# Halo loads in two groups of partitions, low halves in other half steps, and the last two steps in natural order

## The reference

```python
w = np.exp(weight_gen - max); w = w / (sum(w) + 1e-09)          # [B, S, 8, 7]
x_unf = x_pad[:, np.arange(S)[:, None] + np.arange(7)[None, :], :]
out = np.einsum('bshk,bskhg->bshg', w, x_unf)
```

## Time and profile before

| | us |
|---|---|
| median of 3 runs | 1192.06 |
| lowest and highest run | 1190.22, 1192.4 |
| the profiled execution | 1188.5 |
| its span, first to last instruction | 1186.7 |
| PE busy | 1167.5 (98%) |
| DVE busy | 898.3 (76%) |
| ACT busy | 686.6 (58%) |

### The profile page before, as it was taken

The page is one execution under the profiler, slowest core; times in us unless marked ns, Lnnn a source line. Parts: engine busy times, 40 slices in busy tenths (PEclk is TensorE's granted clock), DMA queues, the critical chain, the costliest instruction groups (busy, mean ns, idle before and its releaser), DMA issues.

```text
span 1186.7 us, 26324 instructions
## 1 busy us (share of the span) xinstructions
PE 1167.5 (98%) x10808; PEld 1156.5 (97%) x10808; DVE 898.3 (76%) x998; ACT 686.6 (58%) x802; POOL 3.7 (0%) x11
## 2 busy tenths in 40 slices
PE   6999999999999999999999999999999999999998
PEld 6999999999999999999999999999999999999997
DVE  6888787786877878687786877868678786876564
ACT  5877655556555565555556555565555556555654
POOL 1000000000000000000000000000000000000000
PEclk9999999999999999999999999999999999999999
DMA  8312001010010100000010000100000010000000
GB/s 198 91 44 70 1 18 35 0 50 0 17 33 17 33 0 25 25 17 33 0 50 0 17 33 4 46 0 17 33 17 33 0 50 1 13 1 1 14 1 27
DMA packets 12816, 31.65 MB, mean 27 GB/s; under 512 B 1140, under 2 KB 7666, under 8 KB 12784
## 3 DMA queue, kind: packets, MB, share of 16 engines
q1 hardware_dynamic: 12784, 31.19, 8.4%
HBM read 24.89 MB, written 6.29 MB: 26 GB/s over the span
## 4 chain that ended last, share of the span: by engine, by line
PE 95%; DVE 2%; DMA 1%; ACT 1%; issue 1%; SPq 0%; DVEq 0%; ACTq 0%
PE h_ps L790 44%; PE y_ps L801 30%; PE y_ps L810 20%; PE y_ps L896 1%; DMA stage<-in_moe_w_out_dram 1%; DMA outs<-in_x_dram 1%; DVE acc L527 0%; ACT hid L362 0%; PE y_ps L903 0%; DVE hid_lo L607 0%; PE y_ps L909 0%; DVE prod L549 0%; DVE hid L596 0%; ACT hid L367 0%; ACT wout L349 0%
## 5 line engine op out<-in xcount | busy, mean ns | idle before, releaser
L790 PE MATMUL h_ps<-xt,win 64*128 64x512 f32 (+1 forms) x4860 | 1019.3, 379 | 0.3 <-DVE wout L580 0.3
L790 PEld LDWEIGHTS h_ps<-xt,win 64*128 64x128 f32 x4860 | 803.3, 185 | 0.8 <-DVE wout L580 0.5
L801 PE MATMUL y_ps<-hid_hi,wout 64*128 64x512 f32 (+1 forms) x2160 | 565.9, 381 | 1.3 <-DVE xt L588 1.2
L607 DVE TENSOR_TENSOR hid_lo<-hid,hid_hi 128x1024 fp32r<-128x1024 f32 (+1 forms) x270 | 313.1, 1160 | 173.8 <-ACT hid_hi L378 166.3
L378 ACT ACTIVATE hid_hi<-hid 128x1024 fp32r<-128x1024 f32 (+1 forms) x244 | 256.4, 1051 | 312.4 <-DVE hid L598 143.7
L801 PEld LDWEIGHTS y_ps<-hid_hi,wout 64*128 64x128 f32 x2160 | 370.1, 185 | 8.2 <-DVE xt L588 1.7
L810 PE MATMUL y_ps<-hid_lo,wout 64*128 64x512 f32 (+1 forms) x1080 | 327.5, 383 | 0.0
L801 PE MATMUL y_ps<-hid_lo,wout 64*128 64x512 f32 (+1 forms) x1080 | 322.8, 378 | 2.4 <-DVE hid_lo L607 2.3
L810 PE MATMUL y_ps<-hid_hi,wout 64*128 64x512 f32 (+1 forms) x1080 | 322.5, 378 | 0.0
L801 PEld LDWEIGHTS y_ps<-hid_lo,wout 64*128 64x128 f32 x1080 | 195.2, 185 | 3.0 <-DVE hid_lo L607 2.9
L810 PEld LDWEIGHTS y_ps<-hid_hi,wout 64*128 64x128 f32 x1080 | 195.1, 185 | 0.2
(11 more groups left out here) (70 smaller groups left out, 355.2 us busy)
## 6 DMA issues: line engine op xcount, KB each, us to landing
xwin<-in_x_dram SPq DMA_DIRECT2D x14, 960.0 KB
out_dram<-outs SPq DMA_DIRECT2D x16, 384.0 KB, 2.5
stage<-in_moe_w_out_dram SPq DMA_DIRECT2D x8, 384.0 KB, 6.4
stage<-in_moe_w_in_dram SPq DMA_DIRECT2D x4, 512.0 KB, 6.4
stage<-in_moe_w_in_dram SPq DMA_DIRECT2D x8, 256.0 KB, 6.2
wraw<-in_weight_gen_dram SPq DMA_DIRECT2D x16, 112.0 KB, 2.3
xwin<-in_x_dram SPq DMA_DIRECT2D x1, 768.0 KB
outs<-in_x_dram SPq DMA_DIRECT2D x2, 283.5 KB
```

Of the source, the lines that this page charges most:

```text
L607: dve.tensor_tensor(lo, hid[:, slot, :, 0:width], hi.bitcast(fp32), ALU.subtract).then_inc(lo_done, 1)
L790: return pe.matmul(h_ps[:, s % 2, t, 0:tokens.stop - tokens.start], win[layer][r, wn, cols], src[r, xn, tokens], start=bool(rows) and n in ...
L801: return pe.matmul(ps[:, 0, tokens], wout[layer][r, tile, w_cols], src, start=bool(rows) and s == 0 and n == 0, stop=not rows and s == STE ...
```

## The change

At the start, the halo goes in four loads instead of two: partitions 1 to 48 of each batch, then 49 to 63. SP no longer waits for x's own rows before it issues the weights. PE no longer waits for them before its warm-up, which is 26 matmuls instead of 30. The first two half steps' sums (`hidden_sums`) wait for the parts of x1 one by one, in the order high, low, doubled.

In the half steps, DVE makes `weight_lo(7)` to `weight_lo(10)` one half step later or at another place in it; the layer-2 low halves 12 to 15 move from half steps 23 to 25 to 10, 11, 12 and 16, with their ACT splits two half steps earlier; `softmax_norm(2)` goes from 22 to 23 and `split_x2_lo(0)` from behind half step 21 to 24; the taps of chunk 2 and low halves 16 to 18 are dealt out anew in 24 to 31.

At the end, relu and gate of the last two steps stand in the order of the steps. `output_sums` begins with the products of the high halves and waits for the low halves only then; the sums for the columns above 128 (rest) come before the last ones of the first 128 (main). The last `copy_o` copies cross before main, `add_o` waits for cross alone, and `turn_out` for both.

```diff
@@ -80,7 +80,8 @@
     ALONE = HALVES + STEPS
 
     GATED = range(18, 3 * STEPS)
-    WARM = 30
+    WARM = 26
+    EVEN = 49
...
-            def halo_source(b, halo):
-                return bass.AP(x.tensor, ((b * PB + 1) * ROWS - halo) * D, [[ROWS * D, PB - 1], [1, halo * D]])
+            def halo_source(b, halo, start=1, stop=PB):
+                return bass.AP(x.tensor, ((b * PB + start) * ROWS - halo) * D, [[ROWS * D, stop - start], [1, halo * D]])
 
             def load_first_half():
 
                 sp.dma_start(xwin_first[:, HALO * D:(HALO + JHALF) * D], x_rows[:, 0:JHALF * D]).then_inc(x_own_loaded, 16)
-                for b in range(B):
-                    sp.dma_start(xwin_first[b * PB + 1:(b + 1) * PB, 0:HALO * D],
-                                 halo_source(b, HALO)).then_inc(x_halo_loaded, 16)
+                for start, stop in ((1, EVEN), (EVEN, PB)):
+                    for b in range(B):
+                        sp.dma_start(xwin_first[b * PB + start:b * PB + stop, 0:HALO * D],
+                                     halo_source(b, HALO, start, stop)).then_inc(x_halo_loaded, 16)
...
-            sp.wait_ge(x_own_loaded, 16)
             for n in range(3):
                 load_piece(n)
             load_second_half()
...
-                act.activation(o_main[:, :], ps[:, 0, :], ACT.Copy).then_inc(o_copied, 1)
                 if final:
+                    act.activation(o_cross[:, :], ps[REST:P, 1, :], ACT.Copy).then_inc(o_copied, 1)
                     act.wait_ge(mm2_done, steps + 1)
-                act.activation(o_cross[:, :], ps[REST:P, 1, :], ACT.Copy).then_inc(o_copied, 1)
+                    act.activation(o_main[:, :], ps[:, 0, :], ACT.Copy).then_inc(o_copied, 1)
+                else:
+                    act.activation(o_main[:, :], ps[:, 0, :], ACT.Copy).then_inc(o_copied, 1)
+                    act.activation(o_cross[:, :], ps[REST:P, 1, :], ACT.Copy).then_inc(o_copied, 1)
...
-                if g in (10, 12, 24, 26, 28, 31):
-                    split_piece(PIECES + (10, 12, 24, 26, 28, 31).index(g))
+                if g in (8, 10, 24, 26, 28, 31):
+                    split_piece(PIECES + (8, 10, 24, 26, 28, 31).index(g))
...
             for s in range(STEPS):
-                if s < STEPS - 1:
-                    relu(g0 + s, 1, s % 2)
+                relu(g0 + s, 1, s % 2)
                 if s == 2:
                     copy_o(CHUNKS - 2, g0, y2_ps)
                 if s == 6:
                     copy_out(CHUNKS - 2)
-                    relu(g0 + s + 1, 1, 1 - s % 2)
                 hidden_hi(g0 + s, s % 2, own=s - (STEPS - 2) if s >= STEPS - 2 else None)
...
-                        dve.wait_ge(x_halo_loaded, 16 * B)
+                        dve.wait_ge(x_halo_loaded, 32 * B)
...
-            def add_o(c, ps):
-                dve.wait_ge(o_copied, 2 * c + 2)
+            def add_o(c, ps, final=0):
+                dve.wait_ge(o_copied, 2 * c + 2 - final)
...
                 if g == 1:
                     weight_lo(5)
                     weight_lo(6)
+                if g == 2:
+                    taps(0, [3], 1)
                     weight_lo(7)
-                if 2 <= g < 5:
+                if g in (3, 4):
                     taps(0, [g + 1], 1)
-                    weight_lo(g + 6)
+                    weight_lo(g + 5)
                 if g == 5:
+                    weight_lo(10)
                     taps(0, [6], 1)
...
+                if 10 <= g < 13:
+                    weight_lo(len(LOWS) + g - 10)
...
+                if g == 16:
+                    weight_lo(len(LOWS) + 3)
                 if g == 20:
                     softmax_shift(2)
                 if g == 22:
                     split_x1_lo(1, xt[0], y2_ps, 1)
+                if g == 23:
                     softmax_norm(2)
-                if g == 23:
-                    weight_lo(len(LOWS))
                 if g == 24:
-                    weight_lo(len(LOWS) + 1)
-                    taps(2, [0])
-                if g == 25:
-                    weight_lo(len(LOWS) + 2)
-                    weight_lo(len(LOWS) + 3)
-                if g in (26, 27):
+                    split_x2_lo(0, xt[1])
+                if 25 <= g < 29:
                     taps(2, [g - 25])
-                if g == 28:
+                if g == 29:
                     weight_lo(len(LOWS) + 4)
+                if g == 30:
+                    taps(2, [4])
+                if g == 31:
                     weight_lo(len(LOWS) + 5)
-                if g == 29:
-                    taps(2, [3])
-                if g == 30:
                     weight_lo(len(LOWS) + 6)
-                if g == 31:
-                    taps(2, [4])
                 hidden_lo(g, g % 2, HALF)
                 if g == 18:
                     add_y(0, y2_ps)
-                if g == 21:
-                    split_x2_lo(0, xt[1])
...
-                if s < STEPS - 1:
-                    gate(g0 + s, 1, s % 2)
-                if s == STEPS - 2:
-                    gate(g0 + s + 1, 1, 1 - s % 2)
+                gate(g0 + s, 1, s % 2)
...
-            add_o(CHUNKS - 1, y1_ps)
+            add_o(CHUNKS - 1, y1_ps, final=1)
...
-            def hidden_sums(g, layer, s, src, half):
-
-                _, tokens = whole(half)
-                w = win[layer]
+            def hidden_sums(g, src):
+
+                tiles = [slice((PAIR * g + t) * P, (PAIR * g + t + 1) * P) for t in range(PAIR)]
+                sums = [h_ps[:, g % 2, t, 0:HALF] for t in range(PAIR)]
+                pe.wait_ge(x1_hi, 1)
                 for t in range(PAIR):
-                    cols = slice((PAIR * s + t) * P, (PAIR * s + t + 1) * P)
-                    for n, (wn, xn) in enumerate(LOWER):
-                        ins = pe.matmul(h_ps[:, s % 2, t, 0:tokens.stop - tokens.start], w[:, wn, cols], src[:, xn, tokens],
-                                        start=(n == 0), stop=(n == len(LOWER) - 1))
+                    pe.matmul(sums[t], win[0][:, 0, tiles[t]], src[:, 0, 0:HALF], start=True, stop=False)
+                    pe.matmul(sums[t], win[0][:, 1, tiles[t]], src[:, 0, 0:HALF], start=False, stop=False)
+                pe.wait_ge(x1_lo, 1)
+                for t in range(PAIR):
+                    pe.matmul(sums[t], win[0][:, 0, tiles[t]], src[:, 1, 0:HALF], start=False, stop=False)
+                pe.wait_ge(x1_lo, 2)
+                pe.wait_ge(x1_dup, 1)
+                for t in range(PAIR):
+                    pe.matmul(sums[t], win[0][:, 2, tiles[t]], src[:, 2, 0:HALF], start=False, stop=False)
+                    ins = pe.matmul(sums[t], win[0][:, 3, tiles[t]], src[:, 2, 0:HALF], start=False, stop=True)
                 ins.then_inc(mm1_done, 1)
...
-            def output_sums(g, layer, s, ps, final):
-
+            def output_sums(g, layer, s, ps):
+
+                last = s == STEPS - 1
+                w = wout[layer]
+                his, los = last_hi[s - (STEPS - 2)], last_lo[s - (STEPS - 2)]
+                main, rest = ps[:, 0, :], ps[:, 1, :]
+                tiles = [PAIR * s + t for t in range(PAIR)]
+                pe.wait_ge(hi_done, g + 1)
+                for t, tile in enumerate(tiles):
+                    pe.matmul(main, w[:, tile, HI_MAIN], his[:, t, :], start=False, stop=False)
+                    pe.matmul(main, w[:, tile, LO_MAIN], his[:, t, :], start=False, stop=False)
+                for t, tile in enumerate(tiles):
+                    pe.matmul(rest, w[:, tile, HI_LO_REST], his[:, t, :], start=False, stop=False)
                 pe.wait_ge(lo_done, g + 1)
-                w = wout[layer]
-                his, los = hid_hi[:, s % 2], hid_lo[:, s % 2]
-                if final:
-                    his, los = last_hi[s - (STEPS - 2)], last_lo[s - (STEPS - 2)]
-                main, rest = ps[:, 0, :], ps[:, 1, :]
-                for bank in range(2):
-                    for t in range(PAIR):
-                        tile = PAIR * s + t
-                        hi, lo = his[:, t, :], los[:, t, :]
-                        end = tile == FT - 1
-                        if bank == 0:
-                            pe.matmul(main, w[:, tile, HI_MAIN], hi, start=False, stop=False)
-                            pe.matmul(main, w[:, tile, LO_MAIN], hi, start=False, stop=False)
-                            ins = pe.matmul(main, w[:, tile, HI_MAIN], lo, start=False, stop=end)
-                        else:
-                            pe.matmul(rest, w[:, tile, HI_LO_REST], hi, start=False, stop=False)
-                            ins = pe.matmul(rest, w[:, tile, HI_LO_REST], lo, start=False, stop=end)
-                    if bank == 1 or (final and s == STEPS - 1):
-                        ins.then_inc(mm2_done, 1)
+                for t, tile in enumerate(tiles):
+                    ins = pe.matmul(rest, w[:, tile, HI_LO_REST], los[:, t, :], start=False, stop=last and t == PAIR - 1)
+                if last:
```

(11 more changed lines are left out.)

2 lines of the change are left out of this document (1 added, 1 removed).

## The result

| | before | after |
|---|---|---|
| median | 1191.59 (4 runs, 1190.22 to 1192.4) | 1181.61 (4 runs, 1181.04 to 1182.92) |
| ratio, 95% interval | | 0.9919 [0.9902, 0.9936] |
| the profiled execution | 1188.5 | 1181.4 |
| its span | 1186.7 | 1179.6 |

The change makes the kernel faster by 0.8%. The forecast of 1186.4 (range 1183.5 to 1189.2) had the sign, and was 4.8 us too slow: outside its range. The two profiles differ by 7.1 us where the sum said 5.7. The rest lies between profiles and runs.

A forecast was written before the change was run, and what follows sets the result against it. TensorE's few waits at the start, near 80 us and at the end were taken as the bound; terms 1.8 + 0.5 + 0 + 1.5 + 1.9 = 5.7 us gave a median of 1186.4, range 1183.5 to 1189.2.

The forecast's parts named there:

- What bounds the kernel: Whole span: TensorE waits only a few times, its long waits before 80 us and after 1174 us; edits between win nothing.
- Term 1: Start: halo loads in 48 and 15 rows make weight piece 5 (w_out, tiles 4 to 7) land 1.8 us earlier, bounds 0 to 2.8.
- half of the tail's imbalance: Start, from 25.0 us on: of 1.3 us of idle DMA engines while the last weight pieces land, 0.7 is won.
- Piece 5's own issue is no limit: Start: the issue of piece 5 waits for a low half behind the taps, which come earlier too.
- Term 2: Start, after piece 5 lands: moving weight_lo(7) behind hid_lo brings later steps forward, 0.5 us, bounds 0 and 0.8.
- Term 3: TensorE's own start: earlier first sums and taps are hidden by the weight stream, 0 us, upper bound 0.3.
- Term 4: Middle, near 79 us: x1 low halves and hid_lo made earlier win 1.5 us, bounds 0.9 and 1.7.
- rival (d): Middle: low halves in half steps 10 to 16 make hid_lo late; gain 3.4, 1188.7 us; chance 0.07.
- Term 5: End: natural order of the last steps and cross copied first win 1.9 us, bounds 1.4 and 2.1.
- I carry the gain over unchanged: Whole kernel: the gain summed on the profiled 1188.5 us is applied to the runs' median, 1192.06, 3.6 above it.
- Rival (c): TensorE's clock falls to 0.50 while waiting for piece 5, at most 1.7 us a spell; chance 0.05 (one or two), 0.03 (five).

The follow-up runs named there:

- e1: The kernel before with only the halo loads split into groups of 48 and 15 rows, SyncE's wait kept: 1187.39 us, ratio 0.9975.
- e4: The changed kernel with the halo back in two loads of 63 rows: 1184.73 us, ratio 0.9953 against the kernel before.
- e5: The kernel before with TensorE's start alone changed (26 warm-up matmuls, no wait for x's own rows, staged hidden_sums): 1189.62 us, ratio 0.9992.
- g3: The changed kernel, second window's halo also in 48 and 15 rows, its loads issued behind weight pieces 5 to 7: 1181.04 us, ratio 0.9919.
- h1: The kernel before, unchanged, profiled a second time: 1191.4 us, span 1189.6.
- e2: The kernel before with only SyncE's wait for x's own rows dropped: 1190.57 us, ratio 1.0002.
- i1: The changed kernel with the end of the kernel before: 1183.03 us, ratio 0.9939 against the kernel before.
- e6: The kernel before with the whole end of the change alone: 1188.01 us, ratio 0.9978.
- f2: The kernel before with five useless identity matmuls filling TensorE's pause ahead of the last 20 matmuls: 1188.91 us, ratio 0.9991.

## Why the prediction was off, step by step

**What bounds the kernel.** Right. Each wait named there was won where it was edited, and nothing was won or lost in the loop beyond 0.3 us.

**Term 1, the landing of piece 5: mis-sized.** 3.3 instead of 1.8, above the upper bound of 2.8. The mechanism was the right one in that the row groups decide. The shares went from 0.42 and 0.62 to 1.02 and 1.01, and the groups alone moved the landing by 3.8 in e1 and 2.4 in e4. The traces also count the engines: landings step the halo's semaphore 18 times in the kernel before, 9 for each load of 63 rows, and 62 times in the changed one, 16 and 15 for each batch by the same count. This is the rule that the Trainium skill states (DMA: Bandwidth & Descriptors, "Why a DMA increments its semaphore by 16 and not by 1"), and this trace agrees for 48 and 15 rows too. The row of the same page of the Trainium skill that speaks against two transfers to disjoint parts ("Rules for kernel authors") does not hold here: e1 is such a split alone, and wins 3.8 us of landing. My own reason for 1.8, that 48 is nearer to 64 rows than to 63, is none: 63 is nearer. The wrong step was the pricing. I counted the idle time of the engines, and for the weights I left the 179 GB/s at a share of 1.04 as the speed that the stream would keep. It was full and slow: bytes moved from 6 to 13 us were 1.33 MB before and 2.08 after, at the same share. And the part that I did price, half of the tail's imbalance, was not won at all, since the tail is as before. "Piece 5's own issue is no limit" held (16.39 instead of 18.16).

**Term 2.** 0.47 for 0.5. **Term 3.** 0 for 0; e5 shows it. Once the stream is no longer late it counts: e1, with the old start of TensorE, lost 1.2 of its 3.8 us to ScalarE, and g3, with the new one, could start the split at 21.62 instead of 22.85. No run has the two edits alone together, so that TensorE's start is worth this 1.2 is likely and not isolated. The first tap with halo came at 6.97, not 6.2, because the halo's last part landed only at 6.95.

**Term 4.** 1.9 up to half step 26, 1.6 net, for 1.5; no hid_lo late in half steps 10 to 16 (24.08 and 24.07 between relus 8 and 18), so rival (d) falls. **Term 5.** 1.73 for 1.9. The last 20 matmuls begin 1.34 earlier against the last relu, for 1.44; the rest, 0.39, is as said (0.4), though the transposes wait 0.94 for the main copy. My 1.44 and 0.4 had been rounded up to 1.9.

Together the profiles say 7.1 for 5.7: term 1 is 1.5 over, and the others nearly cancel.

**"I carry the gain over unchanged": wrong, and the larger error.** The changed kernel's runs are 0.2 above its profile, those of before 3.6. So 3.4 of the 4.8 us come from this step: 1.7 because three runs were taken for the level (1192.06, where 90 runs give 1190.4), and 1.7 because the profile of the kernel before was one without a slow stretch in a costly place. The other profiles show those stretches: 1.6 us at the end (h1, e1, e2, i1) and 1.3 to 1.4 in the start (h1, e6). At 4 of 8 and 2 of 6 profiles they make some 1.3 us on average; what makes up the other 0.4 is open. That the pauses bring them is shown for the end as far as counting goes (4 of 8 against 0 of 9); for the early one only two slow cases were seen, and no run isolates it. The timed runs don't settle it: i1 lost 1.4 where the work alone is 1.73, and f2's interval holds 0.

**Rival (c)** had the price of a slow stretch right (at most 1.7) and its sign wrong. It asked whether the clock would fall after the change; the earlier trace rows already showed a pause of 1.3 us ahead of 20 matmuls in the kernel before, and the change removes it.
